# Attention and a mixture of experts on one core: expert rows in groups of up to three tiles, the first layer computed already turned

## The reference

```
logits = x @ w_gate;  expert_idx = argmax(logits, axis=1);  gate_w = softmax(logits)[expert_idx]
disp[e, pos] = x[i]                       # up to capacity = 576 rows for each expert
h = np.maximum(np.einsum('ecd,edf->ecf', disp, w1), 0.0)      # D = 512 -> F = 1024
y = np.einsum('ecf,efd->ecd', h, w2)                          # F = 1024 -> D = 512
out[i] = gate_w[i] * y[expert_idx[i], pos[i]]
```

## Time and profile before

| | us |
|---|---|
| median of 3 runs (lowest, highest) | 414.02 (413.69, 414.33) |
| the profiled execution | 414.16 |
| its span, first to last instruction | 412.5 |
| PE busy | 398.3 |
| DVE busy | 254.8 |
| ACT busy | 200.1 |
| POOL busy | 146.0 |
| mean granted clock of TensorE | 0.993 |

### The profile page before, as it was taken

One profiled execution on the slowest core, in us unless ns is written; L12 is line 12 of the kernel. 1 busy time (PEld: TensorE's weight loads), 2 busy tenths in 40 slices (PEclk: granted clock), 3 DMA queues, 4 the chain that ended last, 5 costly groups with the idle time before them and its releaser, 6 DMA issues.

```text
span 412.5 us, 10630 instructions
## 1 busy us (share of the span) xinstructions
PE 398.3 (97%) x2630; PEld 326.3 (79%) x2631; DVE 254.8 (62%) x802; ACT 200.1 (49%) x530; POOL 146.0 (35%) x228
## 2 busy tenths in 40 slices
PE   7999999999999999999999999999999999999991
PEld 7688888887877777888888888888888888888871
DVE  6787776889798578755566355526755566323220
ACT  2978778877867434555333155223555433122210
POOL 7548888725634423123221123221122221122201
PEclk9999999999999999999999999999999999999997
DMA  9999999999320115656766235706556760111100
GB/s 163 194 294 210 239 235 248 287 229 213 75 78 28 53 27 191 219 207 206 248 226 184 95 107 201 244 25 188 182 197 199 245 216 25 51 51 40 51 25 17
DMA packets 80971, 64.08 MB, mean 155 GB/s; under 512 B 63726, under 2 KB 63726, under 8 KB 80944
## 3 DMA queue, kind: packets, MB, share of 16 engines
q1 hardware_dynamic: 73600, 52.19, 46.4%
q0 software_dynamic: 3520, 10.76, 8.0%
q10 hardware_dynamic: 3824, 0.80, 1.2%
HBM read 54.29 MB, written 10.23 MB: 156 GB/s over the span
## 4 chain that ended last, share of the span: by engine, by line
PE 89%; DVE 4%; SPq 3%; DMA 1%; issue 1%; POOL 0%; ACT 0%; POOLq 0%; DVEq 0%
PE ps L1431 30%; PE ps L1463 18%; PE ps L1467 9%; PE ps L1264 7%; PE ps L1291 7%; PE ps L1451 4%; PE ps L1302 4%; PE ps L1236 4%; PE ps L1272 3%; PE ps L1424 2%; SPq L360 2%; DMA q_rows<-in_q 1%; DVE ps L871 1%; DVE probs L884 1%; PE ps L1348 0%
## 5 line engine op out<-in xcount | busy, mean ns | idle before, releaser
L1431 PE MATMUL ps<-weights_sb,rowsT_hi 128*128 (+1 forms) x336 | 107.8, 402 | 0.0
L809 ACT ACTIVATE hidden<-ps 128x512 f32<-128x512 f32 x20 | 12.0, 598 | 141.4 <-PE ps L1431 89.5
L1463 PE MATMUL ps<-weights_sb,hiddenT_hi 128*128 x320 | 79.2, 390 | 0.5 <-ACT hiddenT_hi L813 0.5
L1168 DVE TENSOR_TENSOR weights_sb<-raw,weights_sb 128x1024 f32 (+1 forms) x56 | 67.1, 1219 | 15.6 <-issue 13.3
L646 POOL DMA_INDIRECT out<-y_sb,dst_now x20 | 20.2, 1008 | 151.5 <-DVE y_sb L1175 151.5
L1431 PEld LDWEIGHTS ps<-weights_sb,rowsT_hi 128*128 128x128 f32 x336 | 61.1, 188 | 13.9 <-issue 0.6
L1463 PEld LDWEIGHTS ps<-weights_sb,hiddenT_hi 128*128 128x128 f32 x320 | 60.0, 188 | 13.3 <-issue 0.7
L1431 PE MATMUL ps<-weights_sb,rowsT_lo 128*128 (+1 forms) x168 | 66.2, 394 | 0.0
L1148 DVE TENSOR_TENSOR hiddenT_lo<-ps,hiddenT_hi 128x512 fp32r<-128x512 f32 x40 | 25.8, 686 | 57.2 <-ACT hiddenT_hi L813 57.2
L798 ACT ACTIVATE weights_sb<-raw 128x1024 f32 (+1 forms) x56 | 56.6, 1068 | 0.0
L696 ACT ACTIVATE probs<-probs,mins 128x128 f32<-128x128 f32 x144 | 55.6, 393 | 0.2 <-DVE mins L884 0.2
(11 more groups left out here) (177 smaller groups left out, 602.2 us busy)
## 6 DMA issues: line engine op xcount, KB each, us to landing
raw<-in_moe_w SPq DMA_DIRECT2D x64, 512.0 KB, 4.1
q_rows<-in_q SPq DMA_DIRECT2D x16, 256.0 KB, 6.0
v_rows<-in_v SPq DMA_DIRECT2D x16, 256.0 KB, 5.7
x_rows<-x_sb SPq DMA_DIRECT2D x16, 256.0 KB, 4.7
k_rows<-in_k SPq DMA_DIRECT2D x14, 256.0 KB, 5.9
k_rows<-in_k ACTq DMA_DIRECT2D x2, 256.0 KB, 7.2
v_rows<-in_v SPq DMA_DIRECT2D x4, 128.0 KB, 6.3
v_front<-in_v SPq DMA_DIRECT2D x4, 128.0 KB, 6.1
```

The source lines that it names most:

```text
L1168: vec.tensor_tensor(weights_sb[:, slot, 2 * layer + 1, part].rearrange("p s n -> p (s n)"), raw[:, j, :], weights_sb[:, slot, 2 * layer, p ...
L1431: ins = te.matmul(dst, left[a], right[c], start=first and n == 0, stop=last and n == 2)
L1463: te.matmul(y_ps(j), hiddenT[0][:, c, :], weights(slot, kind, D * c, D), start=(c == 0 and kind == 2), stop=False)
```

## The change

Rows are taken in groups of up to `SIDE = 3` tiles of one expert. In the first layer the weights are now stationary (128 x 128 blocks of `w1`) and the turned rows of the whole group move, 128 columns for each tile: each of eight chunks of F gives 12 matmuls, and the result `hiddenT_ps` is already turned. So `turn_hidden` and its two splits are gone; ACT makes relu and rounding in one (`relu`), DVE the rest in one (`lower`). The second layer is done chunk by chunk, with the first layer three chunks ahead at the start (`RINGED = 3`), and `turn_rows` of the next group stands behind the second-layer chunks 1, 2 and 3. The group's size and the weights' slot are known when the code is built: PE's loop has one body for every slot and size. A fixed group 0 of two tiles of expert 0 stands ahead of the loop, in straight code. POOL gathers and scatters three tiles in a row in every loop group, absent ones too. The tables count groups instead of tiles.

The core of the diff:

```diff
-            def first_layer_chunks(half, j, slot, chunks):
-                for c in chunks:
-                    at = F * c + 512 * half
-                    last = product(hidden_ps(half), [part[:, c, :] for part in rowsT[j]],
-                                   [weights(slot, kind, at, 512) for kind in (0, 1)], c == 0, c == DC - 1)
-                return last
...
-            def turn_hidden(j):
-                for half in range(2):
-                    for c in range(4):
-                        last = te.transpose(hiddenT_ps(half)[:, c * P:(c + 1) * P],
-                                            hidden[j][:, (4 * half + c) * P:(4 * half + c + 1) * P], ident[:, :])
-                    last.then_inc(hidden_turned, 1)
...
+            def first_layer(n, par, size, slot, c):
+                for d in range(DC):
+                    last = product(hiddenT_ps(c, size), [weights(slot, kind, F * d + P * c, P) for kind in (0, 1)],
+                                   [part[:, d, 0:P * size] for part in rowsT[par]], d == 0, d == DC - 1)
+                last.then_inc(hidden_done, 1)
+
+            def second_layer(n, size, slot, c):
+                pe.wait_ge(hiddenT_ready, n * FC + c + 1)
+                for i in range(size):
+                    last = product(y_ps(i), [part[c % RINGED][:, P * i:P * i + P] for part in hiddenT],
+                                   [weights(slot, kind, D * c, D) for kind in (2, 3)], c == 0, c == FC - 1)
+                    if c == FC - 1:
+                        last.then_inc(y_done[i], 1)
+
+            def group(n, par, size, slot, e):
+                pe.wait_ge(rowsT_ready, all_count(n))
+                pe.wait_ge(w_split[0], e * CHUNKS + CHUNKS)
+                for c in range(RINGED):
+                    first_layer(n, par, size, slot, c)
+                pe.wait_ge(w_split[1], e * CHUNKS + CHUNKS)
+                if not (isinstance(n, int) and n == 0):
+                    pe.wait_ge(y_ready, all_count(n - 1))
+                for c in range(FC):
+                    second_layer(n, size, slot, c)
+                    if c + 2 in TURNED_AT:
+                        turn_rows(n + 1, c + 2 - TURNED_AT[0])
+                    if c + RINGED < FC:
+                        first_layer(n, par, size, slot, c + RINGED)
...
             with pe.Fori(0, PAIRS) as pair:
                 for o in (1, 2):
...
+                    n = pe.snap(pair * 2 + o)
+                    with pe.If(n <= groups):
+                        e = expert_of(n - 1)
+                        size = pe.value_load(size_i[0:1, bass.ds(n - 1, 1)], min_val=0, max_val=SIDE)
+                        slot = pe.snap(e & 1)
+                        for at in range(2):
+                            own = slice(at, at + 1)
+                            with pe.If(slot > 0) if at == 1 else pe.If(slot < 1):
+                                with pe.If(size >= 3):
+                                    group(n, o % 2, 3, own, e)
+                                with pe.If(size < 3):
+                                    with pe.If(size >= 2):
+                                        group(n, o % 2, 2, own, e)
+                                    with pe.If(size < 2):
+                                        group(n, o % 2, 1, own, e)
```

ACT and DVE:

```diff
+            def relu(n, c):
+                size = len(sides(n))
+                act.wait_ge(hidden_done, n * FC + c + 1)
+                nc.scalar.activation(hiddenT[0][c % RINGED][:, 0:P * size], hiddenT_ps(c, size),
+                                     ACT.Relu).then_inc(hiddenT_hi, 1)
...
+            def lower(n, c):
+                size = len(sides(n))
+                dve.wait_ge(hiddenT_hi, n * FC + c + 1)
+                vec.scalar_tensor_tensor(out=hiddenT[1][c % RINGED][:, 0:P * size], in0=hiddenT_ps(c, size), scalar=0.0,
+                                         in1=hiddenT[0][c % RINGED][:, 0:P * size].bitcast(F32),
+                                         op0=ALU.max, op1=ALU.subtract).then_inc(hiddenT_ready, 1)
```

More of the change, by code:

```diff
@@ L343, in head, with tile_count, all_count, sides @@
             return QUAD * quad + [0, 2, 1, 3][n]
+        def tile_count(n, i):
+            return i + 1 if isinstance(n, int) and n == 0 else SIDE * n + i
+        def all_count(n):
+            return SIDE * n + SIDE - 1
+        def sides(n):
+            return range(SIDE - 1 if isinstance(n, int) and n == 0 else SIDE)
         def wait_alone(engine, semaphore, value):
@@ L624, in _ @@
             pool.wait_ge(src_ready, 1)
[L625 to L640, removed]
@@ L853, in _, with split @@
+                    n = act.snap(pair * 2 + o)
+                    with act.If(n <= groups):
+                        due = act.value_load(stage_i[0:1, bass.ds(n - 1, 1)], min_val=0, max_val=E - 1)
+                        def split(layer, j):
+                            with act.If(due > 0):
+                                split_hi(layer, due, j)
+                        group(n, o % 2, split)
         @block.vector
@@ L1185, in _, with group @@
-            vec.tensor_copy(stage_i[:, :], stage[:, :]).then_inc(tables_ready, 1)
-            link(vec.scalar_tensor_tensor(out=is_free[:, :], in0=is_free[:, :], scalar=float(2 * N), in1=src_f[:, :],
-                                          op0=ALU.mult, op1=ALU.add))
-            vec.tensor_copy(dst_row[:, :], is_free[:, :]).then_inc(dst_ready, 1)
-            split_lo(0, 1, 0)
+            def group(n, par, split, after_first=None):
+                for c in range(FC):
+                    lower(n, c)
+                    if c == 0 and after_first:
+                        after_first()
+                    split(c // CHUNKS, c % CHUNKS)
+                    if c in TURNED_AT:
+                        rows_lo(n + 1, 1 - par, c - TURNED_AT[0])
+                    if c == TURNED_AT[-1]:
+                        keep_weights(n + 1, 1 - par)
+                dve.wait_ge(weight_kept, n + 1)
+                if not (isinstance(n, int) and n == 0):
+                    dve.wait_ge(y_free, n)
+                for i in sides(n):
+                    weigh(n, par, i)
@@ L1191, in _ @@
+            for i in range(SIDE - 1):
+                rows_lo(0, 0, i)
+            keep_weights(0, 0)
             dve.wait_ge(first_y_done, 1)
@@ L1229, in _, with split @@
+                    n = dve.snap(pair * 2 + o)
+                    with dve.If(n <= groups):
+                        due = dve.value_load(stage_i[0:1, bass.ds(n - 1, 1)], min_val=0, max_val=E - 1)
+                        def split(layer, j):
+                            with dve.If(due > 0):
+                                split_lo(layer, due, j)
+                        group(n, o % 2, split)
         @block.tensor
@@ L1474, in first_tile_chunks @@
             def first_tile_chunks(half, chunks):
-                return first_layer_chunks(half, 0, slice(0, 1), chunks)
+                for c in chunks:
+                    last = product(first_hidden_ps(half), [part[:, c, :] for part in first_rowsT],
+                                   [weights(slice(0, 1), kind, F * c + 512 * half, 512) for kind in (0, 1)],
+                                   c == 0, c == DC - 1)
+                return last
             def turn_first_hidden(half):
@@ L1485, in first_second_layer @@
                 for c in chunks:
-                    last = product(y_ps(0), [part[:, c, :] for part in first_hiddenT],
+                    last = product(first_y_ps, [part[:, c, :] for part in first_hiddenT],
                                    [weights(slice(0, 1), kind, D * c, D) for kind in (2, 3)], c == 0, c == FC - 1)
```

459 lines of the change are left out of this document (213 added, 246 removed).

## The result

The changed kernel took 484.7 and 487.5 us in its undisturbed runs (of four, 484.69 to 499.71; the other two were disturbed, and ratios leave such runs out here and below) against 413.95 us before (413.69 to 414.33). The ratio is 1.174, with a 95% interval of 1.168 to 1.180: slower. The profiled execution took 484.69 us.

A forecast was written before the change was run, and what follows sets the result against it. PE, busy 97% of the span, was taken to bound the kernel. 414.2 - 8.0 for its work + 45.3 for far jumps net of cover + 8.5 for the clock gave 460 us, eight in ten within 400 to 490.

The forecast's parts named there:

- The work itself, -8.0 us: PE's work with start and tail: transposes saved against first layer, rows, start and tail added, together -8.0 us.
- First layer, +5.9: First layer on PE: 768 matmuls instead of 480, 20 ns paid per matmul beside the columns, +5.9 us.
- the weight load's 188 ns: Rival: in the first layer no step gets below the load's 188 ns, code at hand; 433 us, chance 0.04.
- Hidden transposes -17.4: PE's eight transposes of `hidden` per tile go, 20 x 0.87 us, -17.4 us.
- rows +1.8: PE turns rows of 26 tiles instead of 21, absent ones included, +1.8 us.
- start +0.7: Ahead of group 0: a second hi and lo copy of rows comes behind, partly covered, +0.7 us (0 to 1.3).
- Tail, +1.0: After the last matmuls: three scatters instead of one, the earlier two partly ahead, +1.0 us (0 to 2).
- Sixteen far jumps at 3.3 us: Between PE's loop groups: jumps into code nothing has brought, 16 x 3.3 us, each between 1.1 and 4.4.
- Cover, -7.5: Matmuls still queued on PE hide 1.5 us (0 to 5.4) at each of five transitions with far jumps, -7.5 us.
- Clock, +8.5: PE's clock falls to half in all five gaps; each return costs 1.7 us, +8.5 us.
- Code at hand (406): Rival: PE's loop code is fetched sooner or waited for under the queue; -8.0 us alone, 406 us, chance 0.33.
- Only the back jumps wait (412): Rival: only the three jumps to the start of PE's loop wait, 5.4 us in all; 412 us, chance 0.07.

The follow-up runs named there:

- the straight version: The changed kernel with TensorE's loop written out as seven expert groups, sizes and weight slots constant for these inputs; 402.57 us, 0.972 of the kernel before.
- 5.5-piece loop: The kernel before the change with TensorE's pass written out four times in its loop, three rounds; 414.04 us, 1.0003 of before.
- The loop of 7.8: The changed kernel with the weights' slot tied to group parity, so six bodies in TensorE's loop instead of twelve; 445.03 us, 1.075 of before.
- the loop of 8.3: The kernel before the change with TensorE's pass written out six times in its loop, two rounds; 419.03 us, 1.012 of before.

## Why the prediction was right, and what it mis-sized

The direction and the mechanism held: sixteen far jumps, waiting ahead of the groups of experts 1, 3, 4, 5 and 7, with the clock down behind them. The times, 484.7 and 487.5, lie in the range and 25 or more above the forecast of 460. The account below is of the profiled execution.

- **The work itself, -8.0 us.** Measured in a straight line: 402.4 - 414.2 = -11.8. PE's last matmul ends at 390.1 instead of 403.9, -13.9, and the tail is 2.1 longer (10.6 against 8.6).
- **First layer, +5.9.** Steps of 0.119 and 0.175 us, not 0.127 and 0.180: 4 x 96 x 0.294 = 112.9 us against 112.0, +0.9. The 20 ns a matmul did shrink with the columns, to 12 and 15; the weight load's 188 ns set no floor at these widths, and that rival falls.
- **Hidden transposes -17.4, rows +1.8, second layer 0, start +0.7.** The start's one wait, for `rowsT_lo`, is the 0.7 us in the straight version's row. With the first layer these make -14.0 against the -13.9 measured; one by one they were not measured. Relu, lower halves and splits were covered, as costed at nothing: in the straight version no wait for them is left but that one.
- **Tail, +1.0.** It was +2.1 from the three scatters and what follows them, and 2.8 more from what PE still has to pass behind the last group, which the prediction counted as nothing: two branches of 4.5 and 5.0 us behind the last matmul, the later ones 0.2 (that they go round the same places, as it said, was right for these).
- **Sixteen far jumps at 3.3 us.** The number was exact; each took 4.3, the upper bound (4.4). This is the step that was mis-sized most: 68.7 instead of 52.8 us. Two errors of the count cancel: into expert 5 there were five, not four, since the jump over the body of one tile, taken as free because its target is in the next piece, missed as well; and into expert 4 one of the two took only 1.2 us. That the number came out exact is luck: a jump to the next piece is free only when that piece is already on its way. Into experts 2 and 6 there was a short stall too (idle 1.17 and 0.85, forecast none). q8 brought 48 packets behind 180 us, forecast some forty.
- **Cover, -7.5.** The first jump of a transition was covered for 4.2 us three times, for 2.8 and for 0.2 once, but PE's register loads and the short stalls took as much back: 67.9 us of gaps against 68.7 of far jumps, so a net cover of about 1 us. Gaps: 8.3, 15.7, 4.2, 22.0, 15.7 against the forecast 5.1, 11.7, 5.1, 11.7, 11.7.
- **Clock, +8.5.** 10.7: half of the 21.35 us that PE ran at 1.2 GHz, 2.1 a gap instead of 1.7.
- **The rivals.** Code at hand (406): the straight version is that case, 402.6. Only the back jumps wait (412): they do, but the forward ones too. The jumps' condition, "code that nothing has brought", was right, and the runs sharpen it: brought once is enough only while the loop's pieces stay few.

Sum with measured sizes: 414.2 - 11.8 + 67.9 + 10.7 + 2.8 = 483.8, against 484.7.

## What to carry to other kernels

When a change multiplies the bodies of a loop, count the engine's instructions in the loop and the jumps between pieces of it: up to 5.5 pieces of 16 KB TensorE looped for nothing here, from 7.8 on a missed jump took 3 to 5 us, with a stretch at half the clock behind the gap. Choose between variants by short jumps inside a small loop, or write the groups out in a line; these kept 8.2 to 8.7 us of the 11.4 that the change is worth in straight code, and that the twelve bodies had turned into a loss of over 70. An engine's idle time put down to "issue" together with many q8 packets is the sign of it, and the cheapest test is to write that engine's loop out.

## What the runs showed of the hardware that was not expected

- Code stays held over several pieces: the back jump of a 5.5-piece loop fetched nothing. The Trainium skill, page "Runtime: NRT & Kernel Launch", section "Instruction fetch mechanics", has a taken branch wait whenever its target is outside a window of two pages; these runs differ, and the measurement decides. The same section's other figure, 128 KiB for TensorE filled in blocks of 16 KiB, would be eight pieces, and agrees with 5.5 held and 8.3 not. The loop of 7.8, somewhat under eight, missed too; a loop that begins within a piece touches one more (q8 brought eight pieces beside the one at hand in the first round of the loop of 8.3), but no run lies between 5.5 and 7.8.
- A miss takes 3.0 to 5.3 us, against 1.1 us that a packet took by the queue's share. A jump whose piece is already on its way takes 1.2 to 1.6 us.
- A pair of weight load and matmul has a step of 0.119 us at 256 columns, though the load's record lasts 188 ns.
- With a hint at the head of each pass a kernel of 445 us took 17.8 less; two of three back jumps went from 4.6 to 0.2 us, the third did not.
